# Small routing tables in bfloat16 instead of float32, and the first one-hot columns made in two halves

## The chip, the core and the metric

The kernel runs on one NeuronCore of one Trainium2 chip. The metric is the device time of one execution in microseconds (us), the median over several executions.

## The reference

Three stages follow each other, all on float32 data.

```python
# 1. retention attention: q, k, v of shape (4, 8, 768, 64)
gamma = 1.0 - 2.0 ** (-5.0 - np.arange(H))
for t in range(S):
    state = gamma[None, :, None, None] * state + np.einsum('bhd,bhe->bhde', k[:, :, t], v[:, :, t])
    y[:, :, t] = scale * np.einsum('bhd,bhde->bhe', q[:, :, t], state)
x = y.transpose(0, 2, 1, 3).reshape(3072, 512)

# 2. mixture of 8 experts, each takes exactly 384 tokens
logits = x @ w_gate                            # (3072, 8)
order = np.argsort(-logits.flatten())          # all (token, expert) pairs, highest first
for idx in order:
    tok, e = int(idx) // E, int(idx) % E
    if assigned[tok] >= 0 or counts[e] >= cap: continue
    assigned[tok] = e
    counts[e] += 1
out[mask] = np.maximum(x[mask] @ w1[e], 0.0) @ w2[e]     # for each e, mask = assigned == e

# 3. gated layer with d_ff = 1536
gate = 1.0 / (1.0 + np.exp(-(x @ w_gate2)))
return gate * (x @ w_val) @ w_out
```

## The kernel before, in words

**The order of the work.** The attention runs first, over 24 units of 128 tokens (`attend_*`, 0 to about 131 us). In the same time SyncE (SP) loads q, k and v, stores the finished rows to a buffer `xrows` in DRAM, and begins to load the weights of the third stage that stay in SBUF (`resident`). Each matrix product of stages 2 and 3 is made of three float32r products (high x high, high x low, low x high), so each weight piece is split in a high part (ScalarE) and a low part (VectorE or GpSimd) before use.

**The routing.** It assigns tokens to experts without a sort. Each partition holds 24 tokens (U = 24) and 8 experts (E = 8), so a table over both has 192 columns. VectorE (the DVE) takes for each token its best open expert (`prepare_keys`, `prepare_digits`: `best`, `wide`, `top`, `choice`), turns the logit into an integer key of 7 digits of 5 bits, and then finds digit by digit the key down to which the fullest expert is filled. Every step is a "visit": VectorE writes a small table, TensorE multiplies it with a table of ones or a triangle to sum over partitions, and VectorE reads the sum back (`route(vis, i)` on VectorE, `visit(vis, i)` on TensorE). Visits 1 to 7 are digits (`compare_first`, L981, in the first round; `compare`, L991, in the others). `V_TIE` (L1080 to L1088) counts ties, `V_COUNT` (L1091 to L1101) says which of them fit, `V_RANK` (L1104 to L1117) finds the filled expert and its members, `V_IDS` (L1121 to L1124) their ranks. `make_onehot` (L1133, L1135) writes for each token a one-hot row `onehot` (32 columns by the low rank bits) and a row `slot_ids` (24 columns) that carries the token's number in the block of its rank. TensorE multiplies them (L1355, 24 matmuls in the first round), which turns them into the list of token numbers, `route_ids` (L1163) writes it to `ids`, and GpSimd gathers the 384 rows of x from DRAM (L839) in three thirds.

**Tables and how they are read.** The two operands of an operation on a 192-column table come as `[P, E, U]`. `per_token(ap)` repeats a 24-column table over the experts (the outer dimension has step 0, the inner one has step 1); `per_expert(ap)` repeats an 8-column table over the tokens (the inner dimension has step 0). `over_experts(ap)` turns the order to `[P, U, E]`, so a reduction over the inner dimension steps by 24 elements.

**Which of the routing is in the open.** The routing for the first expert, round 0, stands alone between the attention and the first expert's products: nothing else is left for TensorE. All instructions of VectorE follow each other there (`link` makes the next one wait for the last). After the first ids `close` and `prepare(False)` begin the second routing, then VectorE splits 4 weight pieces of `ring` (L1211) and the low part of x (L1192). TensorE runs 44 matmuls without use (`keep_busy`, L1367) while the gather is under way, transposes x (L1375), and the main loop begins with L1382. The routing of round i + 1 is laid into the products of round i: TensorE's visits are put by a planner at given columns of the product stream, and VectorE's steps between its other duties.

**Queues.** SP issues all plain transfers in the order of the program: in the attention q, k, v, 4 stores and, now and then, a resident weight; later the late resident weights; after `expert_id` is known (L1113) the 8 ring pieces of the expert (L784). GpSimd issues the gathers (L839) and the final scatters (L853).

**Places in SBUF.** The tables are laid one behind the other in the order of their declaration, each starting at a multiple of 32 bytes in the partition. Behind them comes `resident` at byte 29696, and behind that `ring`, `xh`, `xl`, `hh`, `hl`, `h2h`, `h2l`. The tiles of the attention (`qraw` at byte 115712, `kraw`, `vraw`, `xrow`, ...) are laid over these and move with them. The loads into `qraw`, `kraw` and `vraw` write runs of 256 bytes (64 floats), those into a resident or ring piece of w1, w2, w_gate or w_val runs of 512 bytes.

Of the kernel before, what the change touches and what calls it, by code (L numbers as in the profile page):

```python
# [4 lines left out]
F32 = mybir.dt.float32  # L5
F32R = mybir.dt.float32r
BF16 = mybir.dt.bfloat16
# [3 lines left out]
ALU = mybir.AluOpType  # L11
ACT = mybir.ActivationFunctionType
AX_X = mybir.AxisListType.X
P = 128

def retention_moe_glu_kernel(nc, q, k, v, w_router, w1, w2, w_gate, w_val, w_out, decay, out):
    B, H, S, D = q.shape
    E = w_router.shape[1]
    C = S // P  # L20
    U = B * C
# [11 lines left out]
    with ctx:  # L33
        def sb(name, shape, dt):
            return ctx.enter_context(nc.sbuf_tensor(name, shape, dt))

        def sem(name):
            return ctx.enter_context(nc.semaphore(name))
# [32 lines left out]
        EVACUATED = KF + KD  # L71
# [7 lines left out]
        QUAD = 32  # L79
        QUADS = P // QUAD  # L80
        BLOCKS = CAP // QUAD
# [40 lines left out]
        tied = sb("tied", [P, E, U], BF16)  # L122
        tied_before = sb("tied_before", [P, E, U], BF16)
        fresh = sb("fresh", [P, E, U], BF16)
        wide = sb("wide", [P, E, U], F32)
        best = sb("best", [P, U], F32)
        top = sb("top", [P, 2, U], F32)
        bits = sb("bits", [P, U], F32)
        key = sb("key", [P, U], I32)
        digit_f = sb("digit_f", [P, DIGITS, U], BF16)  # L130
        prefix = sb("prefix", [P, U], BF16)
        is_above = sb("is_above", [P, U], F32)
        is_on = sb("is_on", [P, U], F32)
        fits = sb("fits", [P, U], F32)
        taken = sb("taken", [P, U], F32)
        member = sb("member", [P, U], BF16)
        members_to = sb("members_to", [P, U], F32)
# [2 lines left out]
        rank_low = sb("rank_low", [P, U], I32)  # L140
        rank_block = sb("rank_block", [P, U], I32)
        in_block = sb("in_block", [P, U, BLOCKS], BF16)
        member_id = sb("member_id", [P, U, 2], BF16)
        slot_ids = sb("slot_ids", [P, U, 2, BLOCKS], BF16)
        slot_sums = sb("slot_sums", [P, 2 * BLOCKS], F32)
        room = sb("room", [P, E], F32)
        limit = sb("limit", [P, E], F32)
        filled = sb("filled", [P, E], F32)
        closing = sb("closing", [P, E], F32)
        keeping = sb("keeping", [P, E], F32)  # L150
        numbered = sb("numbered", [P, E], F32)
# [16 lines left out]
        raised = sb("raised", [P, U], F32)  # L168
        shift = sb("shift", [P, DIGITS], I32)
        expert_iota = sb("expert_iota", [P, E], F32)  # L170
        priority = sb("priority", [P, E], F32)
        column = sb("column", [P, QUAD], F32)
        block_iota = sb("block_iota", [P, BLOCKS], F32)
        position = sb("position", [P, U, 2], F32)
# [23 lines left out]
        def placed(name, shape, dt, offset):  # L198
            return nc.alloc_sbuf_tensor_at(name, shape, dt, offset=offset)
# [12 lines left out]
        onehot = placed("onehot", [P, U, QUAD], BF16, at_hl + TT * DM * 4)  # L212
# [14 lines left out]
        onehot_ready = sem("onehot_ready")  # L227
# [22 lines left out]
        h_done = sem("h_done")  # L250
# [697 lines left out]
        def _(dve):  # L948
# [176 lines left out]
                                                 block_iota[:, :].unsqueeze(1).to_broadcast([P, U, BLOCKS]), ALU.is_equal))  # L1125

            def make_onehot(i):
                if not (isinstance(i, int) and i == 0):
                    dve.wait_ge(h_done, EVACUATED * i)
                if isinstance(i, int) and i == 0:  # L1130
                    for c in range(C):
                        dve.wait_ge(xrow_stored[c], STORED * (B + 1))
                nc.vector.tensor_tensor(onehot[:, :, :], column[:, :].unsqueeze(1).to_broadcast([P, U, QUAD]),  # L1133
                                                   rank_low[:, :].unsqueeze(2).to_broadcast([P, U, QUAD]), ALU.is_equal).then_inc(onehot_ready, 1)
                nc.vector.tensor_tensor(slot_ids[:, :, :, :], in_block[:, :, :].unsqueeze(2).to_broadcast([P, U, 2, BLOCKS]),  # L1135
                                        member_id[:, :, :].unsqueeze(3).to_broadcast([P, U, 2, BLOCKS]), ALU.mult).then_inc(onehot_ready, 1)

            def close():

# [172 lines left out]
        def _(pe):  # L1312
# [4 lines left out]
            def visit(vis, i):  # L1317
                if vis < V_TIE:

                    for t in range(0, U, FOLD):  # L1320
                        if t == 0:
                            pe.wait_ge(half_compared, i * DIGITS + vis + 1)
                        if t == U // 2:
                            pe.wait_ge(route_ready, i * (VISITS - 1) + vis + 1)
                        if isinstance(i, int) and i == 0:
                            bins = above_first[:, t // FOLD, :, :].rearrange("p r t -> p (r t)")
                        else:
                            bins = above[:, t:t + FOLD, :].rearrange("p t r -> p (t r)")
                        last = nc.tensor.matmul(PS_R[:, 0:FOLD * E], bins, choice[:, :, t:t + FOLD], start=t == 0, stop=t == U - FOLD)  # L1329
                    last.then_inc(route_done, 1)  # L1330
                    if isinstance(i, int) and i == 0:
                        pe.wait_ge(partial_ready, vis + 1)
                        for t in range(FOLD):
                            last = nc.tensor.matmul(PS_K[:, 0:E], fold[:, t, :, :].rearrange("p k r -> p (k r)"), partial[:, :, t],
                                                    start=t == 0, stop=t == FOLD - 1)
                        last.then_inc(folded, 1)
                    return
                if vis < V_IDS:
                    pe.wait_ge(route_ready, i * (VISITS - 1) + vis + 1)
                if vis == V_TIE:  # L1340

                    nc.tensor.matmul(PS_R[:, 0:NF], below[:, :], tied[:, :, :].rearrange("p e u -> p (e u)"), start=True, stop=False)
                    nc.tensor.matmul(PS_R[:, 0:NF], ones[:, :], tied_before[:, :, :].rearrange("p e u -> p (e u)"), start=False, stop=True)
                    last = nc.tensor.matmul(PS_K[:, 0:E], ones[:, :], counted[:, :], start=True, stop=True)
                elif vis == V_COUNT:
                    last = nc.tensor.matmul(PS_K[:, 0:E], ones[:, :], counted_fresh[:, :], start=True, stop=True)
                elif vis == V_RANK:

                    nc.tensor.matmul(PS_K[:, 0:U], below[:, :], member[:, :], start=True, stop=False)
                    last = nc.tensor.matmul(PS_K[:, 0:U], ones[:, :], members_before[:, :], start=False, stop=True)  # L1350
                else:
                    pe.wait_ge(onehot_ready, 2 * (i + 1))
                    if isinstance(i, int) and i == 0:
                        for t in range(U):
                            last = nc.tensor.matmul(PS_R[0:QUAD, 0:2 * BLOCKS], onehot[:, t, :],  # L1355
                                                    slot_ids[:, t, :, :].rearrange("p n m -> p (n m)"), start=t == 0, stop=t == U - 1)
                    else:
                        for t in range(0, U, QUADS):
                            last = nc.tensor.matmul(PS_R[:, 0:QUADS * 2 * BLOCKS], onehot[:, t:t + QUADS, :].rearrange("p t c -> p (t c)"),
                                                    slot_ids[:, t:t + QUADS, :, :].rearrange("p t n m -> p (t n m)"),  # L1360
                                                    start=t == 0, stop=t == U - QUADS)
                last.then_inc(route_done, 1)
# [170 lines left out]
```

## Time and profile before

| | us |
|---|---|
| median of 3 executions | 1074.85 (1074.79 to 1075.24) |
| the profiled execution | 1075.28 |
| its span | 1073.5 |
| TensorE busy (matmuls) | 1029.4 (96%) |
| VectorE busy | 704.0 (66%) |
| ScalarE busy | 326.2 (30%) |
| GpSimd busy | 122.6 (11%) |
| mean granted TensorE clock | 0.979 |

The span is the time from the first to the last recorded instruction or transfer of the profiled execution; 1.8 us lie around it. Busy shares are averages over stages with different limits, so they have to be read by stage: the attention (0 to 131 us), the routing of the first expert in the open (131 to 174 us), the main loop (174 to 1062 us) and the last rows on their way out (1062 to 1073.5 us).

### The profile page before, as it was taken

What the parts mean: (1) busy time and instruction counts of PE and PEld (TensorE: products, weight loads), DVE (VectorE), ACT (ScalarE), POOL (GpSimd) and SP (SyncE); (2) the same over time, 40 slices, a digit from 0 to 9 for tenths busy, and PEclk for the clock granted to TensorE, in tenths of its full rate; (3) what the DMA queues carried; (4) which work ended last, traced back from release to release, by engine and by line L of the source; (5) the groups of instructions that cost most, each with busy time, mean ns of one, the idle gap of its engine ahead of it and who ended that gap; (6) DMA issues with size and microseconds to landing.
All of it is one profiled execution on the core that took longest, in us unless ns stands there. A gap on an engine that the chain in (4) does not pass through costs nothing.

```text
span 1073.5 us, 20171 instructions
## 1 busy us (share of the span) xinstructions
PE 1029.4 (96%) x7186; PEld 960.5 (89%) x7186; DVE 704.0 (66%) x1880; ACT 326.2 (30%) x622; POOL 122.6 (11%) x149
## 2 busy tenths in 40 slices
PE   8999728999999999999999999999999999999995
PEld 7888618989999999999999999999999999999995
DVE  4777778788678657765776577667765677554211
ACT  3222144412342234223332333223322341334110
POOL 4323301045200110010101010001001100110001
PEclk9999958999999999999999999999999999999998
DMA  9989765304230414132413232233214231423000
GB/s 204 211 211 224 170 201 155 111 4 140 77 116 21 128 55 134 39 89 79 131 58 89 79 119 70 61 106 109 80 48 120 89 99 40 128 70 117 2 1 29
DMA packets 197356, 107.69 MB, mean 100 GB/s; under 512 B 81936, under 2 KB 182800, under 8 KB 197264
## 3 DMA queue, kind: packets, MB, share of 16 engines
q1 hardware_dynamic: 193424, 93.94, 31.6%
q0 software_dynamic: 3840, 12.59, 3.7%
q8 instruction: 50, 0.82, 0.3%
q14 instruction: 42, 0.34, 0.1%
HBM read 88.41 MB, written 18.09 MB: 99 GB/s over the span
## 4 chain that ended last, share of the span: by engine, by line
PE 95%; DVE 3%; issue 1%; DMA 1%; POOL 0%; DVEq 0%; ACT 0%; POOLq 0%
PE bank L1382 21%; PE bank L1384 21%; PE bank L1383 21%; PE bank L1475 6%; PE bank L1476 6%; PE bank L1474 6%; PE bank L660 2%; PE bank L730 2%; PE bank L726 2%; PE bank L686 1%; PE bank L1329 1%; PE bank L693 1%; PE bank L740 1%; PE bank L638 1%; PE bank L707 1%
## 5 line engine op out<-in xcount | busy, mean ns | idle before, releaser
L1382 PE MATMUL bank<-h2h,resident 128*128 128x384 f32 x768 | 261.2, 340 | 0.0
L1384 PE MATMUL bank<-h2h,resident 128*128 128x384 f32 x768 | 257.9, 336 | 0.0
L1383 PE MATMUL bank<-h2l,resident 128*128 128x384 f32 x768 | 257.3, 335 | 0.0
L1382 PEld LDWEIGHTS bank<-h2h,resident 128*128 128x128 f32 x768 | 144.3, 188 | 2.9
L1383 PEld LDWEIGHTS bank<-h2l,resident 128*128 128x128 f32 x768 | 144.3, 188 | 2.9
L1384 PEld LDWEIGHTS bank<-h2h,resident 128*128 128x128 f32 x768 | 144.1, 188 | 0.0
L885 ACT ACTIVATE ring<-ring_raw 128x512 fp32r<-128x512 f32 x192 | 117.7, 623 | 54.7 <-DMA ring_raw<-in_moe_w_out_dram 43.1
L1202 DVE TENSOR_TENSOR pf<-bank,gate 128x384 f32<-128x384 f32 x96 | 53.5, 557 | 116.0 <-PE bank L1384 108.1
L1211 DVE TENSOR_TENSOR ring<-ring_raw,ring 128x512 fp32r<-128x512 f32 x192 | 128.7, 696 | 0.0
L909 ACT ACTIVATE ph<-pf 128x384 fp32r<-128x384 f32 x96 | 50.4, 525 | 257.5 <-DVE pf L1202 257.5
L1206 DVE TENSOR_TENSOR pl<-pf,ph 128x384 fp32r<-128x384 f32 x96 | 55.4, 577 | 56.8 <-ACT ph L909 56.8
L905 ACT ACTIVATE gate<-bank 128x384 f32<-128x384 f32 x96 | 46.9, 489 | 141.2 <-PE bank L1384 141.1
L1382 PE MATMUL bank<-xh,ring 128*128 128x384 f32 x256 | 87.6, 342 | 0.9 <-DVE xl L1192 0.9
L1382 PE MATMUL bank<-hh,ring 128*128 128x384 f32 x256 | 87.0, 340 | 0.0
L1384 PE MATMUL bank<-xh,ring 128*128 128x384 f32 x256 | 85.7, 335 | 0.0
L1383 PE MATMUL bank<-hl,ring 128*128 128x384 f32 x256 | 85.7, 335 | 0.0
L1384 PE MATMUL bank<-hh,ring 128*128 128x384 f32 x256 | 85.7, 335 | 0.0
L1383 PE MATMUL bank<-xl,ring 128*128 128x384 f32 x256 | 85.7, 335 | 0.0
L1476 PE MATMUL bank<-ring,pl 128*128 128x512 f32 x192 | 76.0, 396 | 0.0
L1475 PE MATMUL bank<-ring,ph 128*128 128x512 f32 x192 | 75.8, 395 | 0.0
L839 POOL DMA_INDIRECT xg<-xrows,ids x24 | 23.7, 989 | 455.4 <-DVE ids L1163 417.2
L1474 PE MATMUL bank<-ring,ph 128*128 128x512 f32 x192 | 74.8, 390 | 0.2 <-issue 0.2
(195 smaller groups left out, 1660.2 us busy)
## 6 DMA issues: line engine op xcount, KB each, us to landing
ring_raw<-in_moe_w_dram SPq DMA_DIRECT2D x128, 256.0 KB, 3.1
ring_raw<-in_moe_w_out_dram SPq DMA_DIRECT2D x64, 256.0 KB, 2.9
qraw<-in_q_dram SPq DMA_DIRECT2D x24, 256.0 KB, 4.1
kraw<-in_k_dram SPq DMA_DIRECT2D x24, 256.0 KB, 4.3
vraw<-in_v_dram SPq DMA_DIRECT2D x24, 256.0 KB, 4.4
xrows<-xrow SPq DMA_DIRECT2D x96, 64.0 KB, 2.1
xlaid<-xg SPq DMA_DIRECT2D x7, 768.0 KB, 4.5
zg<-xlaid SPq DMA_DIRECT2D x28, 192.0 KB, 4.2
```

Of the source, the lines that this page charges most:

```text
L885: nc.scalar.activation(ring[:, n % RING, 0, :], ring_raw[n % RING][:, :], ACT.Copy).then_inc(piece_hi, 1)
L905: nc.scalar.activation(gate[:, f % 2, :], bank[2 * (f % 2)][:, 0:CAP], ACT.Sigmoid).then_inc(gate_ready, 1)
L909: nc.scalar.activation(ph[:, f % 2, :], pf[:, f % 2, :], ACT.Copy).then_inc(ph_ready, 1)
L1202: nc.vector.tensor_tensor(pf[:, f % 2, :], bank[2 * (f % 2) + 1][:, 0:CAP], gate[:, f % 2, :], ALU.mult).then_inc(p_ready, 1)
L1206: nc.vector.tensor_tensor(pl[:, f % 2, :], pf[:, f % 2, :], ph[:, f % 2, :].bitcast(F32), ALU.subtract).then_inc(pl_ready, 1)
L1211: nc.vector.tensor_tensor(ring[:, s, 1, :], ring_raw[s][:, :], ring[:, s, 0, :].bitcast(F32), ALU.subtract).then_inc(piece_lo, 1)
L1382: nc.tensor.matmul(ps, wh, xhi, start=start, stop=False)
L1383: nc.tensor.matmul(ps, wh, xlo, start=False, stop=False)
L1384: return nc.tensor.matmul(ps, wl, xhi, start=False, stop=stop)
L1474: nc.tensor.matmul(PS_OUT[j][:, :], ph[:, f % 2, toks], wh, start=f == 0, stop=False)
L1475: nc.tensor.matmul(PS_OUT[j][:, :], ph[:, f % 2, toks], wl, start=False, stop=False)
L1476: last = nc.tensor.matmul(PS_OUT[j][:, :], pl[:, f % 2, toks], wh, start=False, stop=False)
```

## The change

Seven tables change their type from float32 to bfloat16: `wide` (192 columns), `top` (48), `is_above`, `is_on`, `fits` (24 each), `filled` and `priority` (8 each). All of them hold whole numbers up to 24 (flags, priorities 8 to 1, counts up to 24), which bfloat16 holds exactly. `make_onehot` of the first round (`i == 0`) writes tokens 0 to 11 and then tokens 12 to 23, each half with its own pair of instructions and its own increments of `onehot_ready`; TensorE starts its first 12 matmuls after the first pair and waits again before the 13th. For the other rounds the instructions are as before, and the count that TensorE waits for is 2 higher, since the first round now increments four times.

```diff
@@ -122,16 +122,16 @@
         tied = sb("tied", [P, E, U], BF16)
         tied_before = sb("tied_before", [P, E, U], BF16)
         fresh = sb("fresh", [P, E, U], BF16)
-        wide = sb("wide", [P, E, U], F32)
+        wide = sb("wide", [P, E, U], BF16)
         best = sb("best", [P, U], F32)
-        top = sb("top", [P, 2, U], F32)
+        top = sb("top", [P, 2, U], BF16)
         bits = sb("bits", [P, U], F32)
         key = sb("key", [P, U], I32)
         digit_f = sb("digit_f", [P, DIGITS, U], BF16)
         prefix = sb("prefix", [P, U], BF16)
-        is_above = sb("is_above", [P, U], F32)
-        is_on = sb("is_on", [P, U], F32)
-        fits = sb("fits", [P, U], F32)
+        is_above = sb("is_above", [P, U], BF16)
+        is_on = sb("is_on", [P, U], BF16)
+        fits = sb("fits", [P, U], BF16)
         taken = sb("taken", [P, U], F32)
         member = sb("member", [P, U], BF16)
         members_to = sb("members_to", [P, U], F32)
@@ -145,7 +145,7 @@
         slot_sums = sb("slot_sums", [P, 2 * BLOCKS], F32)
         room = sb("room", [P, E], F32)
         limit = sb("limit", [P, E], F32)
-        filled = sb("filled", [P, E], F32)
+        filled = sb("filled", [P, E], BF16)
         closing = sb("closing", [P, E], F32)
         keeping = sb("keeping", [P, E], F32)
         numbered = sb("numbered", [P, E], F32)
@@ -168,7 +168,7 @@
         raised = sb("raised", [P, U], F32)
         shift = sb("shift", [P, DIGITS], I32)
         expert_iota = sb("expert_iota", [P, E], F32)
-        priority = sb("priority", [P, E], F32)
+        priority = sb("priority", [P, E], BF16)
         column = sb("column", [P, QUAD], F32)
         block_iota = sb("block_iota", [P, BLOCKS], F32)
         position = sb("position", [P, U, 2], F32)
@@ -1125,15 +1125,20 @@
                                                  block_iota[:, :].unsqueeze(1).to_broadcast([P, U, BLOCKS]), ALU.is_equal))
 
             def make_onehot(i):
-                if not (isinstance(i, int) and i == 0):
-                    dve.wait_ge(h_done, EVACUATED * i)
                 if isinstance(i, int) and i == 0:
                     for c in range(C):
                         dve.wait_ge(xrow_stored[c], STORED * (B + 1))
-                nc.vector.tensor_tensor(onehot[:, :, :], column[:, :].unsqueeze(1).to_broadcast([P, U, QUAD]),
-                                                   rank_low[:, :].unsqueeze(2).to_broadcast([P, U, QUAD]), ALU.is_equal).then_inc(onehot_ready, 1)
-                nc.vector.tensor_tensor(slot_ids[:, :, :, :], in_block[:, :, :].unsqueeze(2).to_broadcast([P, U, 2, BLOCKS]),
-                                        member_id[:, :, :].unsqueeze(3).to_broadcast([P, U, 2, BLOCKS]), ALU.mult).then_inc(onehot_ready, 1)
+                    parts = 2
+                else:
+                    dve.wait_ge(h_done, EVACUATED * i)
+                    parts = 1
+                n = U // parts
+                for part in range(parts):
+                    tiles = slice(part * n, part * n + n)
+                    nc.vector.tensor_tensor(onehot[:, tiles, :], column[:, :].unsqueeze(1).to_broadcast([P, n, QUAD]),
+                                            rank_low[:, tiles].unsqueeze(2).to_broadcast([P, n, QUAD]), ALU.is_equal).then_inc(onehot_ready, 1)
+                    nc.vector.tensor_tensor(slot_ids[:, tiles, :, :], in_block[:, tiles, :].unsqueeze(2).to_broadcast([P, n, 2, BLOCKS]),
+                                            member_id[:, tiles, :].unsqueeze(3).to_broadcast([P, n, 2, BLOCKS]), ALU.mult).then_inc(onehot_ready, 1)
 
             def close():
 
@@ -1349,9 +1354,11 @@
                     nc.tensor.matmul(PS_K[:, 0:U], below[:, :], member[:, :], start=True, stop=False)
                     last = nc.tensor.matmul(PS_K[:, 0:U], ones[:, :], members_before[:, :], start=False, stop=True)
                 else:
-                    pe.wait_ge(onehot_ready, 2 * (i + 1))
+                    pe.wait_ge(onehot_ready, 2 if i == 0 else 2 * (i + 2))
                     if isinstance(i, int) and i == 0:
                         for t in range(U):
+                            if t == U // 2:
+                                pe.wait_ge(onehot_ready, 4)
                             last = nc.tensor.matmul(PS_R[0:QUAD, 0:2 * BLOCKS], onehot[:, t, :],
                                                     slot_ids[:, t, :, :].rearrange("p n m -> p (n m)"), start=t == 0, stop=t == U - 1)
                     else:
```

By the rule of 32 bytes, `wide` takes 384 bytes less in a partition, `top` 96 less, `is_above`, `is_on` and `fits` 32 less each (48 bytes are rounded to 64), `filled` and `priority` nothing less. Everything behind them, from `resident` on, starts 576 bytes earlier.

## Rows read from the trace of the kernel before

**Rows 1.** The chain that ended last, its shares of the span by engine.

```profile
PE 95%; DVE 3%; issue 1%; DMA 1%; POOL 0%; DVEq 0%; ACT 0%; POOLq 0%
```

**Rows 2.** Stretches: length; PE, PEld, DVE, ACT, POOL busy; granted clock; DMA share; GB/s.

```profile
80.50:107.00 26.50, 26.50 (x416) 23.13 (x414) 21.05 (x39) 7.42 (x18) 8.70 (x9) 1.00 0.96 226
...
167.00:168.00 1.00, 1.00 (x8) 0.95 (x7) 0.93 (x5) 0.72 (x2) 0.70 (x1) 0.50 1.11 334
...
600.00:800.00 200.00, 200.00 (x1165) 188.81 (x1164) 137.01 (x393) 63.53 (x118) 8.99 (x10) 1.00 0.28 84
```

**Rows 3.** What TensorE waited for from 176 us on: us, times, longest.

```profile
PE bank L1474 <- issue: 0.2, 1, 0.2
```

**Rows 4.** Timeline, first routing: start us, us, engine, line, operation, shapes, [idle before].

```profile
133.48 0.61 DVE L1043 TENSOR_REDUCE top<-wide 128x24 f32<-128x192 f32 x1
...
152.41 0.36 DVE L1082 TENSOR_TENSOR tied<-choice,is_on 128x192 bf16<-128x192 bf16 x1
...
153.28 0.33 DVE L1085 TENSOR_TENSOR strict<-choice,is_above 128x192 bf16<-128x192 bf16 x1
...
153.65 0.35 DVE L1087 TENSOR_REDUCE counted<-strict 128x8 bf16<-128x192 bf16 x1
153.92 0.35 DVE L1088 TENSOR_TENSOR tied_before<-wide,tied 128x192 bf16<-128x192 f32 x1
...
155.46 0.62 DVE L1094 TENSOR_REDUCE fits<-wide 128x24 f32<-128x192 f32 x1
156.11 0.36 DVE L1095 TENSOR_TENSOR fresh<-tied,fits 128x192 bf16<-128x192 bf16 x1
156.50 0.26 DVE L1096 TENSOR_TENSOR fresh<-fresh,strict 128x192 bf16<-128x192 bf16 x1
...
157.35 0.48 DVE L1100 TENSOR_REDUCE taken<-fresh 128x24 f32<-128x192 bf16 x1
...
159.03 0.61 DVE L1109 TENSOR_REDUCE member<-wide 128x24 bf16<-128x192 f32 x1
159.67 0.15 DVE L1113 CAST expert_id<-expert_f 128x1 int32<-128x1 f32 x1
...
161.24 4.94 SPq L784 DMA_DIRECT2D ring_raw<-in_moe_w_dram  x8
161.49 0.96 DVE L1133 TENSOR_TENSOR onehot<-column,rank_low 128x768 bf16<-128x768 f32 x1
162.36 0.75 DVE L1135 TENSOR_TENSOR slot_ids<-in_block,member_id 128x576 bf16<-128x576 bf16 x1
163.17 0.81 PE L1355 MATMUL bank<-slot_ids,onehot 128*32 128x24 bf16 x24 [2.73 <-DVE slot_ids L1135]
```

**Rows 5.** Groups by line and form, DVE: xcount, busy us, mean ns, idle before.

```profile
L991 DVE TENSOR_TENSOR above<-prefix,ladder 128x384 bf16<-128x384 bf16 x84 | 43.2, 555 | 1.5
...
L981 DVE TENSOR_TENSOR above_first<-prefix,ladder 128x384 bf16<-128x384 bf16 x12 | 3.8, 355 | 0.2
```

**Rows 6.** The chain from the ids to the main loop: start us, us, what.

```profile
165.76 4.95 DMA xg<-xrows,ids
...
173.18 0.50 ACT xh L890
...
173.71 0.57 DVE xl L1192
```

**Rows 7.** Timeline: first load of the attention, then k of the last unit.

```profile
1.25 0.42 SPq L376 DMA_DIRECT2D qraw<-in_q_dram  x1
...
111.12 1.04 POOL L480 TENSOR_TENSOR ks<-kraw,dec 128x512 f32<-128x512 f32 x1 [0.63 <-DMA kraw<-in_k_dram]
...
115.77 0.60 PE L693 MATMUL bank<-ident,ks 128*128 128x128 f32 x4
```

**Rows 8.** Timeline beside the gather: `keep_busy` and the splits of four weight pieces.

```profile
163.91 6.29 PE L1367 MATMUL bank<-segment,ones 128*128 128x192 bf16 x44
...
170.76 2.49 DVE L1211 TENSOR_TENSOR ring<-ring_raw,ring 128x512 fp32r<-128x512 f32 x4
```

## The prediction, made before the changed kernel was run

> **What bounds the kernel now.** I read the chain of waits first. TensorE holds 95% of the chain that ended last, VectorE 3% [rows 1]. The stretches say where each applies: in the attention TensorE is busy for the whole of 26.5 us, in the main loop for 200 of 200 us [rows 2]. The waits confirm the loop: from 176 us on TensorE waited 0.2 us in all [rows 3]. VectorE is busy for 137 of 200 us there [rows 2], and none of its routing ends late. So whatever the change saves in the routings of the seven later experts is worth nothing, and it must be judged on the routing of the first one, which lies in the open between the attention and L1382.
>
> The timeline of that stretch is a single line of VectorE instructions, each waiting for the last, with short visits to TensorE between them [rows 4]. There a nanosecond off an instruction is a nanosecond off the start of the main loop, as long as nothing else becomes late. From the ids on the chain is the gather (4.95 us from the first issue to landing), the transposes, ScalarE's `xh` and VectorE's `xl` [rows 6].
>
> **Part 1, element by element.** Which of the tables gain is read from three rows. `fresh <- fresh,strict`, all bfloat16 with inner step 1, takes 0.26 us for 192 columns; `fresh <- tied,fits`, the same but for a float32 `fits`, takes 0.36 [rows 4]. `tied_before`, with one float32 operand, takes 0.35. So one float32 operand costs the fast rate. What a step of 0 does is seen in the two compares of 384 columns: `above_first`, whose inner run has step 1 and whose step of 0 lies further out, takes 355 ns, and `above`, whose inner step on an operand is 0, takes 555 ns [rows 5]. A table repeated over the outer dimension keeps the fast rate, one repeated over the inner does not.
>
> In the changed kernel `tied` and `strict` (through `per_token`), `tied_before` and `fresh <- tied,fits` become all bfloat16 with inner step 1. I set each at 0.26 us: `tied` 0.36 to 0.26, `strict` 0.33 to 0.26, `tied_before` 0.35 to 0.26, `fresh` 0.36 to 0.26 [rows 4]. Sum 0.10 + 0.07 + 0.09 + 0.10 = 0.36 us. Lower bound 0.09 (only `tied_before`, where nothing is repeated), if the repetition over the experts does spoil the rate; upper bound 0.40. The other writes of `wide` keep a float32 operand or a PSUM source, or they use `per_expert` (`priority`, `filled`) with inner step 0: nothing. `is_on`, `is_above` and `filled` are of 24 and 8 columns, where the fixed part is nearly all of the time: nothing, at most 0.02 us each either way. The scan that writes `wide` goes column after column already on bfloat16 operands: nothing.
>
> **Part 2, reductions.** `top`, `fits` and `member` reduce `wide` over the experts, stepping by 24 elements, in 0.61, 0.62 and 0.61 us. `taken` reduces a bfloat16 table in the same order in 0.48 us, and `counted` reduces as many columns with step 1 in 0.35 us [rows 4]. `taken` is an addition and the three are a maximum and a minimum, so the 0.13 us between them may be the type (a step of 48 bytes in place of 96) or the operation. I take the type, since maximum and minimum agree with each other and the step is what divides `counted` from `taken`: 0.13 + 0.14 + 0.13 = 0.40 us. Bounds: 0 if it is the operation; 0.26 + 0.27 + 0.26 = 0.79 if they fell to `counted`.
>
> The Trainium skill ("VectorE: DVE Perf Modes", The perf-mode tier table) puts `tensor_reduce` at one element per cycle for bfloat16 and float32 alike. Taken alone that gives the reductions nothing and a whole change of 0.6 us in place of 1.0. The rows do show reductions of 192 columns at 0.35, 0.48 and 0.61 us, so something beside the count of columns sets their time here.
>
> **Part 3, the two halves.** Before: `onehot` starts at 161.49, `slot_ids` at 162.36, that is 0.87 us later for 768 columns, and ends at 163.11; TensorE starts at 163.17 and needs 0.81 us for 24 matmuls [rows 4]. The slope is (0.96 - 0.555) / 384, about 1.05 ns a column, from `onehot` and from `above` with 384 columns [rows 4, 5], so 0.40 us for 384 columns and 0.80 for 768, with 0.155 fixed, of which 0.07 remain when the next instruction needs no wait (0.87 - 0.80). Two halves then start at 161.49, 161.49 + 0.40 + 0.07 = 161.96, + 0.30 + 0.07 = 162.33, + 0.47 = 162.80, and the last ends after 0.30 + 0.15 at 163.25. TensorE's first 12 matmuls start at 162.47 and are over near 162.9, hidden under VectorE's second half. The other 12 start at 163.31 and take 0.43 us (half of 0.81 and a little for the start), to 163.74, where it was 163.98 before. Gain 0.24 us. The half costs VectorE 0.14 us (two more instructions) and saves 0.38 on TensorE. The bounds are -0.14 (the matmuls pass nothing on) and 0.38 (the extra instructions cost nothing). The second wait stands ahead of matmul 13; behind it are the last matmuls and `keep_busy`, which nobody waits for.
>
> **Sum and what is late next.** Up to `expert_id` the chain shortens by 0.36 + 0.40 = 0.76 us, up to the ids by 1.00 us. Behind that:
> - SP issues the 8 ring pieces after `expert_id` (161.24 before, so 160.5) and GpSimd the gather after the ids (165.76, so 164.8). Both use the transfer engines, which are full while they run (share 1.11 at 334 GB/s in [rows 2]). The gather moves 1.00 us, the pieces that it competes with only 0.76. Its landing should move by something between; I take 0.9.
> - `keep_busy` ended at 163.91 + 6.29 = 170.20, 0.5 us before the first third was there (170.71) [rows 6, 8]. It moves by 1.0 too, so it stays in cover, and TensorE's granted clock (0.50 in [rows 2], the level of 1.2 GHz) rises as far into it as before.
> - VectorE's four splits ended at 170.76 + 2.49 = 173.25, and `xh` was there at 173.68 [rows 6, 8]: 0.43 us of slack. They move by 1.0 and by another 0.13 from `top` in the second preparation.
>
> So 0.9 us. The profiled execution took 1075.28 us, 1.8 more than its span of 1073.5, and 0.43 more than the median. It becomes 1074.4, and the median 1074.85 becomes **1073.95 us**. All three parts without loss in the gather give 1073.85; with the upper bounds of parts 1 and 2 and 0.24 for the halves 1.43, hence 1073.4.
>
> **Edits of place.** Everything from `resident` on starts 576 bytes earlier. It began at a multiple of 512 and will begin 448 past one, so each 256-byte run of q, k and v that was written from a multiple of 256 begins 192 past one. No row of before shows loads with such a start. Cost taken: nothing; the bound on the bad side is the third rival.
>
> **Rivals.**
> 1. *The type does little.* The step of 0 keeps `tied`, `strict` and `fresh` at one rate and the reductions are slow by their operation. Left are `tied_before` and the halves, 0.09 + 0.24 = 0.33 us: 1074.5. For it: no row shows `per_token` on all-bfloat16 operands, and `taken` differs in its operation. Against it: `above_first` at 355 ns.
> 2. *The gather is bound by the transfers in front of it.* Then its landing moves with the pieces only, 0.76 us: 1074.1. For it: the full share of 1.11. Against it: the first third is the first of three to ask for its bandwidth and gets it beside the pieces.
> 3. *Slower: the loads of the attention take longer at their new places.* The place is k of the last unit. It landed at 111.12, GpSimd was done with it at 112.16, and TensorE took it at 115.77 [rows 7]: 3.6 us of slack, the end of loads that SP began to issue at 1.25 us [rows 7] and that share the engines at 0.96 [rows 2]. Loads longer by more than 3.6 / 109.9 = 3.3% make TensorE wait. If they took 10% longer, the attention would end 11.0 - 3.6 = 7.4 us later, less the 0.9: 1081.3. For it: the share of 0.96, and that the slack is only 3% of the stretch. Against it: TensorE never waited for these loads before, and the bytes are the same.
>
> **How the numbers follow.** Forecast (0.6 to 1.3 us, the second rival inside it, of which it has 0.2): 0.67. First rival: 0.14. Third: 0.08. A gain of over 2.15 us by the new places, which I can't derive: 0.05. Something else within 0.2%: 0.06. What a measurement of this kernel tells from no change is about 0.2%, 2.15 us, 1072.7 to 1077.0. The forecast, both small rivals and the rest lie inside, so faster 0.05, same 0.86, slower 0.09. The range of 8 in 10 takes the forecast, the first rival and a part of the rest: 1073.0 to 1075.4.
>
> **What the new profile would show.** `tied`, `strict`, `tied_before` and `fresh <- tied,fits` at 0.26 us; `top`, `fits` and `member` near 0.48 (at 0.61 part 2 is wrong, and the operation was the cause); `onehot` and `slot_ids` twice at about 0.55 and 0.45, L1355 in two groups of 12, the second ending about 2.25 us after the first `onehot` began (2.49 before); `expert_id` 0.76 us and L1382 0.9 us earlier against the end of the attention. The end of the attention unmoved says that the third rival is out. The forecast fails if TensorE waits for `ks` or `qraw` before 120 us, or if the main loop, from L1382 to the last L1466, differs in length by more than 0.3 us.

## The result and the profile after

The changed kernel is slower. Its median over 19 executions is 1077.13 us (1075.58 to 1078.92), that of the kernel before, run beside it, 1075.21 (1074.28 to 1076.17). The ratio is 1.0018, 95% interval 1.0012 to 1.0024. The forecast was 1073.95 with a range up to 1075.4. What the change does to instructions came out close to the forecast; the loss came from where the large tiles lie. The profiled execution took 1078.59 us, its span is 1076.8, 3.3 more than that of before.

The timeline of the first routing after the change (columns as in [rows 4]):

```profile
133.89 0.47 DVE L1043 TENSOR_REDUCE top<-wide 128x24 bf16<-128x192 bf16 x1
...
152.66 0.26 DVE L1082 TENSOR_TENSOR tied<-choice,is_on 128x192 bf16<-128x192 bf16 x1
...
153.43 0.23 DVE L1085 TENSOR_TENSOR strict<-choice,is_above 128x192 bf16<-128x192 bf16 x1
...
153.97 0.25 DVE L1088 TENSOR_TENSOR tied_before<-wide,tied 128x192 bf16<-128x192 bf16 x1
...
155.41 0.48 DVE L1094 TENSOR_REDUCE fits<-wide 128x24 bf16<-128x192 bf16 x1
155.92 0.26 DVE L1095 TENSOR_TENSOR fresh<-tied,fits 128x192 bf16<-128x192 bf16 x1
...
158.73 0.47 DVE L1109 TENSOR_REDUCE member<-wide 128x24 bf16<-128x192 bf16 x1
...
161.05 0.56 DVE L1138 TENSOR_TENSOR onehot<-column,rank_low 128x384 bf16<-128x384 f32 x1
...
162.36 0.45 DVE L1140 TENSOR_TENSOR slot_ids<-in_block,member_id 128x288 bf16<-128x288 bf16 x1
162.87 0.50 PE L1362 MATMUL bank<-slot_ids,onehot 128*32 128x24 bf16 x12 [0.34 <-DVE slot_ids L1140]
163.30 5.17 PE L1374 MATMUL bank<-segment,ones 128*128 128x192 bf16 x44
```

Each of these lines answers to one of [rows 4] and is about as short as forecast; only L1362's second group took 0.50 us where 0.43 was forecast. From the start of `best` (131.63 before, 132.19 after) to the first gather (165.76 and 165.16) VectorE's chain took 34.13 us before and 32.97 after, 1.16 us less. Of these, 0.14 us are not the change's: `bits` took 0.32 us in the profile of before, where it ran beside a subtraction on GpSimd, and 0.18 us here. That leaves 1.02 us, for 1.00 forecast.

What came against it stands in three other views. First the stretch from 5 to 105 us (columns as in [rows 2]) of before, and then of after:

```profile
5.00:105.00 100.00, 100.00 (x1547) 88.04 (x1543) 71.91 (x127) 27.59 (x63) 33.78 (x49) 1.00 0.94 218
```

```profile
5.00:105.00 100.00, 98.48 (x1540) 86.36 (x1538) 71.62 (x126) 27.72 (x63) 33.82 (x49) 1.00 1.05 215
```

And the transfers of the hardware queue over the whole span (packets, MB, share of 16 engines' time), of before and of after:

```profile
q1 hardware_dynamic: 193424, 93.94, 31.6%
```

```profile
q1 hardware_dynamic: 193424, 93.94, 33.8%
```

Same packets and bytes, more engine time: per packet 0.316 x 16 x 1073.5 / 193,424 = 28.1 ns before and 30.1 ns after, and in the attention a share of 1.05 for 215 GB/s where 0.94 carried 218, 13% more time a byte. TensorE, never idle there before, now waits. Second, that wait, in the timeline of after:

```profile
9.89 1.04 POOL L480 TENSOR_TENSOR ks<-kraw,dec 128x512 f32<-128x512 f32 x1 [2.94 <-DMA kraw<-in_k_dram]
...
10.99 0.66 PE L693 MATMUL bank<-ident,ks 128*128 128x128 f32 x4 [1.28 <-POOL ks L480]
...
112.15 1.04 POOL L480 TENSOR_TENSOR ks<-kraw,dec 128x512 f32<-128x512 f32 x1 [0.47 <-DMA kraw<-in_k_dram]
...
116.33 0.60 PE L693 MATMUL bank<-ident,ks 128*128 128x128 f32 x4
```

These are the longest wait, at the second unit, and k of the last unit. The start of the attention in before (the first 48 matmuls, then k of the second and of the third unit), and then in after (the 48 matmuls, k of the third and of the fourth unit):

```profile
2.92 5.39 PE L638 MATMUL bank<-ident,dec 128*64 128x128 f32 x48 [2.92 <-DMA dec<-in_decay_dram]
...
10.95 0.60 PE L693 MATMUL bank<-ident,ks 128*128 128x128 f32 x4
...
14.09 0.60 PE L693 MATMUL bank<-ident,ks 128*128 128x128 f32 x4
```

```profile
2.85 4.23 PE L638 MATMUL bank<-ident,dec 128*64 128x128 f32 x48 [2.85 <-DMA dec<-in_decay_dram]
...
14.59 0.66 PE L693 MATMUL bank<-ident,ks 128*128 128x128 f32 x4 [0.24 <-POOL ks L480]
...
19.28 0.60 PE L693 MATMUL bank<-ident,ks 128*128 128x128 f32 x4
```

The wait of 1.28 us is not what is lost. TensorE takes k of the second unit at 10.99 us, at 10.95 in before; it stood ready earlier, because its first 48 matmuls took 4.23 us in this execution and 5.39 in the other. The loss comes right behind: the third unit is 0.50 us later than before (14.59 for 14.09), the fourth 0.56 (19.28 for 18.72), and it stays 0.56 to the last. At the last unit 3.1 us of slack are left, nearly the 3.6 of [rows 7]. Third, the gather in the chain of waits (start us, us), then TensorE's timeline behind it, then the stretches by the microsecond:

```profile
165.16 6.40 DMA xg<-xrows,ids
```

```profile
171.60 0.75 PE L1382 MATMUL bank<-ident,xg 128*128 128x128 f32 x4 [3.13 <-DMA xg<-xrows,ids]
...
175.99 0.66 PE L1389 MATMUL bank<-xh,ring 128*128 128x384 f32 x1 [0.62 <-DVE xl L1197]
```

```profile
170.00:171.00 1.00, 0.00 (x0) 0.00 (x0) 1.00 (x4) 0.73 (x2) 0.00 (x0) 1.00 1.06 388
...
173.00:174.00 1.00, 1.00 (x8) 0.91 (x8) 0.00 (x0) 0.00 (x0) 0.00 (x0) 0.50 0.00 0
...
178.00:179.00 1.00, 1.00 (x9) 0.95 (x9) 1.00 (x3) 0.00 (x0) 0.00 (x0) 0.50 0.08 16
```

The gather lands 6.40 us after its issue, 4.95 before [rows 6]. TensorE had run out of `keep_busy` at 168.47 and idled for 3.13 us (0.56 before); some 1.5 us after it resumed the granted clock was at 0.50 (1.2 GHz), and stayed there past 178 us.

The 3.3 us of span add up by these marks: end of the attention +0.56, VectorE's chain -1.16, issue of the gather to the first transpose +1.44, from there to the first product +0.74 (3.65 to 4.39, half the clock), main loop +1.68 (887.75 to 889.43 between the first product and the last `orow`, half the clock at its start), tail +0.04.

### The profile page after: what moved, and what is told of

It reads as the page before. It is cut to its first block, busy times and chain, and to the rows that moved or that the text cites. A ratio compares the mean times of both kernels' runs of the same rounds, so it can differ in the third digit from the quotient of the medians.

```text
span 1076.8 us, 20173 instructions
## 1 busy us (share of the span) xinstructions
PE 1030.3 (96%) x7186; PEld 960.7 (89%) x7186; DVE 697.5 (65%) x1882; ACT 326.7 (30%) x622; POOL 122.3 (11%) x149
## 3 DMA queue, kind: packets, MB, share of 16 engines
q1 hardware_dynamic: 193424, 93.94, 33.8%
## 4 chain that ended last, share of the span: by engine, by line
PE 94%; DVE 3%; DMA 1%; issue 1%; SPq 1%; POOL 0%; DVEq 0%; ACT 0%; POOLq 0%
PE bank L1389 21%; PE bank L1391 21%; PE bank L1390 21%; PE bank L1482 6%; PE bank L1483 6%; PE bank L1481 6%; PE bank L660 2%; PE bank L730 2%; PE bank L726 2%; PE bank L1334 1%; PE bank L686 1%; PE bank L693 1%; PE bank L740 1%; PE bank L707 1%; DMA xg<-xrows,ids 1%
```

## The experiments

Theory P: the 576 bytes that the smaller tables free shift every large tile off a multiple of 256 bytes, and the transfers that write or read them take longer. Rivals: C, the halves start TensorE earlier and `keep_busy` no longer covers the gather; B, the bfloat16 tables cost something themselves. Every comparison is with the kernel before, run on the same chip (medians 1075.21 to 1075.28).

**The places alone.** To the changed kernel, or to the kernel before, one unused table is added behind the small ones:

```diff
+        room_left = sb("room_left", [P, 16], F32)    # a_even: changed kernel, resident at 29184, a multiple of 512
+        room_left = sb("room_left", [P, 112], F32)   # b_odd: kernel before, resident at 30144, 448 past one
         at_above = nc.sbuf_base
```

> The changed kernel with 64 unused bytes behind the tables, so that resident and everything behind it begin at a multiple of 512 bytes again (29184), as in the kernel before (29696); after has 29120. Theory P (places): the slower kernel comes from transfers that write and read tiles at 448 past a multiple of 512. Then the transfer share of the hardware queue falls from 33.8% back to 31.6%, TensorE no longer waits for ks (1.5 us in after), the first third of the gather lands about 5.0 us after its issue (6.4 in after), and the time is 1073.8 to 1074.6, 1.2 to 0.6 under before. Theory C (cover): the first half of the one-hot columns starts TensorE 1.1 us earlier, its clock rises earlier, the 44 keep_busy matmuls run out in 5.2 instead of 6.3 us, TensorE idles and its clock falls before the main loop. Then the gap and the fall stay in part of the executions whatever the places: some of them at about 1073.9 and others at about 1076. Theory B (bfloat16 tables cost something by themselves): the time stays at 1077.

> The kernel before with 448 unused bytes behind the tables: no other edit, all large tiles begin 448 past a multiple of 512, as in after. Theory P: transfer share of the hardware queue near 33.8% (31.6 before), TensorE waits 0.5 to 1.5 us for ks in the attention, the gather's first third lands 6 us after its issue instead of 5, so TensorE idles some 1.5 us behind keep_busy instead of 0.6, and the time is 1.0 to 3.5 us above before. Theory C or B: as before, within 0.3 us.

a_even: 1074.41 us (11 executions, 1073.49 to 1077.59), ratio 0.9995 (0.9986 to 1.0004). b_odd: 1077.94 us (8, 1076.86 to 1079.02), ratio 1.0026 (1.0015 to 1.0036). The same stretch and the gather in the chain, first of a_even (hardware queue 31.8%), then of b_odd (33.8%):

```profile
5.00:105.00 100.00, 100.00 (x1550) 88.02 (x1547) 72.53 (x128) 27.46 (x63) 34.80 (x50) 1.00 0.95 220
```

```profile
164.05 5.25 DMA xg<-xrows,ids
```

```profile
5.00:105.00 100.00, 99.53 (x1538) 87.26 (x1536) 71.44 (x126) 27.59 (x63) 33.87 (x49) 1.00 1.04 213
```

```profile
166.39 6.23 DMA xg<-xrows,ids
```

With no other edit, the kernel before becomes 2.7 us slower by an unused table, with the share and the gather of after and a wait for `ks` of 0.5 us (1.5 in after). The changed kernel is brought from 1.9 us over before to 0.8 under it. P holds; B falls. That a_even is faster than before is not shown by its times, since the interval includes 1.

In the profile of b_odd the clock did not fall (1.00 from 169 to 180 us), though TensorE was idle for 2.42 us ahead of the transposes:

```profile
172.66 0.75 PE L1376 MATMUL bank<-ident,xg 128*128 128x128 f32 x4 [2.42 <-DMA xg<-xrows,ids]
```

So it shows the cost of the places without the clock. Its span is 2.2 us longer than that of before: end of the attention +0.54, VectorE's chain +0.09, issue of the gather to the first transpose +1.27 (6.27 for 5.00), from there to the first product nothing (3.65), main loop +0.23 (887.98 for 887.75), tail +0.07.

**The two edits apart**, both with the tiles at a multiple of 512:

```diff
-                    parts = 2       # types_even: the changed tables and 64 unused bytes, one-hot columns in one piece
+                    parts = 1
-        wide = sb("wide", [P, E, U], BF16)   # halves_only: wide and the six other tables in float32
+        wide = sb("wide", [P, E, U], F32)
```

> The seven tables in bfloat16, one-hot columns in one piece as before, large tiles at a multiple of 512. By the durations seen in after (best to expert_id) 0.9 us less VectorE time ahead of the gather; keep_busy starts with the ids as before, so TensorE idles no longer than before. All theories but B: 0.6 to 0.9 us under before, and no spread wider than that of before. B: slower than before.

> Only the first one-hot columns in two halves, tables in float32, places as before. The ids come 0.25 us earlier. Theory C: TensorE starts 0.7 us earlier, the clock may rise a step earlier and keep_busy ends up to 1.3 us earlier, so that TensorE idles 1 to 2 us ahead of the first transposes and the clock falls in some executions: the times lie in two groups about 2.4 us apart, the lower 0.25 us under before. Theory P or B: 0.2 us under before, in one group.

types_even: 1074.22 us (1073.81 to 1077.13), 1.0 under before, ratio 0.9993 (0.9984 to 1.0002). halves_only: 1075.15 (1074.83 to 1075.64), ratio 1.0000 (0.9991 to 1.0009). A gain of 0.2 us is less than these intervals can tell; none shows, and types_even without the halves is no slower than a_even with them (1074.41). In the profile of halves_only the first gather was issued 33.80 us after `best` began, 0.33 earlier than before (0.14 of it is `bits` again), and the first transpose came 5.39 us after that, 0.39 later than before. This is what my second rival would give, but it is not shown: the same stretch took 5.42 us in b_256 (below), which has the gather, the instructions and the alignment of before, so that it moves as much from one execution to the next. C as I put it falls: `keep_busy` took 6.29 us in halves_only, as before, and 4.96 in types_even, where the halves are not. When the clock rises in it differs from one execution to the next.

**The fall of the clock.** The changed kernel with its tiles misplaced, and with them in place, with a longer cover:

```diff
-            keep_busy(44)
+            keep_busy(60)     # a_busy60: places of the changed kernel
+            keep_busy(50)     # a_even_busy50: with the 64 unused bytes of a_even
```

> The changed kernel with its tiles where they are (448 past a multiple of 512), keep_busy(60) in place of keep_busy(44). The profile of after has TensorE idle for 3.1 us between keep_busy and the first third of x, then the granted clock at 0.5 from about 173 to 178 us, which costs some 2.4 us against before in the transposes and the first products. The 19 times of after lie between 1075.6 and 1078.9, 8 of them under 1076.5. Theory D (the fall of the clock behind a gap is what spreads them, on top of the places): without the gap all times lie at 1075.6 to 1076.6, median 1076.1. Theory E (the spread is that of the transfers alone): median and spread as in after, 1077.1 and 1075.6 to 1078.9.

> The changed kernel with 64 unused bytes behind the tables and keep_busy(50) in place of 44: both costs taken away. Expected 1074.2 to 1074.4, 0.8 to 1.0 under before, and no time at 1077 (a_even had one at 1077.6 in 11). If the longer keep_busy itself runs past the landing of x, 1074.6 to 1075.0.

a_busy60: 1076.04 us (1075.71 to 1077.18), ratio 1.0008 (0.9999 to 1.0017); its granted clock was 1.00 from 171 to 180 us. Of the 19 times of the changed kernel 10 are above 1077, of these 11 one. That one is the profiled execution, in which the clock did not fall. So the longer cover takes most of the slow executions away, 1.1 us between the medians (1077.13 - 1076.04). How much of this is the clock's fall is not shown. In the profile of after it cost 2.4 us (0.74 + 1.68 above). Its 6.6 us at half the clock take 0.003 off the mean granted clock of an execution, which is 0.982 at the most in any run. Of the ten executions above 1077 four have a mean of 0.978 and two of 0.979, but four have 0.980 or 0.981, which hardly leaves room for such a fall, and the median one (1077.13, 0.980) is one of these. By this the clock fell in some six of 19 at the most, and something else makes others slow. Nor does every gap bring a fall: in the profiles it came behind gaps of 3.13 us (after) and 2.49 (a_attn_even, below), and not behind 2.44 (b_32), 2.42 (b_odd), 2.16 (b_64) and 2.14 (types_even). What is left in a_busy60, 0.8 us over before, is at the edge of what these executions tell from nothing. a_even_busy50: 1074.12 (1073.85 to 1075.10), ratio 0.9993 (0.9984 to 1.0002), without the single time at 1077 that a_even and types_even had.

**Which tiles.** Only the attention's tiles moved back, or only ring and what lies behind it:

```diff
-        shared = at_big + (RESIDENT - SHARED) * 2 * 512 * 4
+        shared = at_big + (RESIDENT - SHARED) * 2 * 512 * 4 + 64   # a_attn_even
+        room_left = sb("room_left", [P, 16], F32)                  # a_ring_even
         at_ring = nc.sbuf_base
```

> The changed kernel with only the tiles of the attention moved 64 bytes on, so that qraw, kraw and vraw begin at a multiple of 512; resident, ring and xg stay at 448 past one. Theory F (the place costs mostly in the attention): the attention ends as before, TensorE does not wait for ks, and the time is near that of a_even, 1074.4 to 1075.0. Theory G (it costs mostly in the first round, where resident, ring and gather share the engines): the share of the attention falls to that of before, the gather still lands in 6 us and the time is 1076 to 1077.

> The changed kernel with 64 unused bytes between resident and ring: ring, xg and all behind them begin at a multiple of 512; resident and the tiles of the attention stay at 448 past one. Theory F: the attention still ends some 0.5 us late and the time stays above 1076. Theory G: the first third of the gather lands within 5.2 us, the times lie at 1074.6 to 1075.2 and are no more spread than those of before.

a_attn_even: 1075.29 us (1074.47 to 1077.57), ratio 1.0002 (0.9993 to 1.0011). The share from 5 to 105 us is 0.95 at 221 GB/s, TensorE does not wait for `ks`, but the first transpose follows the gather's issue by 5.81 us, and in 2 of 11 the time is over 1077. a_ring_even: 1074.83 (1073.17 to 1076.92), ratio 0.9995 (0.9986 to 1.0004). Its share is 1.05 at 216 GB/s and it waits for `ks`; that stretch takes 5.34 us. Each half cures its own stage, so both theories are half right; the 5.81 us of a_attn_even lie between the 5.00 to 5.53 of the kernels with every tile in place and the 6.15 to 6.44 of those with none, so the attention's tiles may have a part in the gather too.

The wait for `ks` alone is a poor sign of the places: a_even_busy50 and a_split_busy50 (below) wait 0.74 and 0.76 us at the second unit with the attention's tiles in place, and their first 48 matmuls took 4.14 and 4.34 us. What goes with the places in all profiles is the time from k of the second unit to k of the third on TensorE: 3.60 to 3.62 us in the six kernels with the attention's tiles off a multiple of 256, 3.13 to 3.20 in the eight with them on one. TensorE took k of the last unit at 116.17 to 116.43 us in the six and at 115.05 to 115.77 in the eight.

Two things were not expected. GpSimd's last split of a resident weight ran into the first routing (it began at 131.37 us in after, behind loads that landed earlier); timeline of a_ring_even:

```profile
132.88 1.27 POOL L279 TENSOR_TENSOR resident<-resident_raw,resident 128x512 fp32r<-128x512 f32 x1
132.94 1.43 DVE L1035 TENSOR_TENSOR wide<-logits,best 128x192 bf16<-128x192 f32 x1
```

VectorE's 0.35 us instruction takes 1.43 and ends 0.2 us after GpSimd's. A like hold stands in the profiles of a_busy60 and b_64, where `key` takes 1.12 us in place of 0.18, and not in that of after. And the rounds of the main loop were shorter in a_ring_even than in any kernel so far. The start of `orow` in two rounds that follow each other, first a_even, then a_ring_even:

```profile
507.26 1.89 DVE L1223 COPY orow<-bank 128x512 f32<-128x512 f32 x3 [1.96 <-PE bank L1474]
618.56 1.89 DVE L1223 COPY orow<-bank 128x512 f32<-128x512 f32 x3 [1.96 <-PE bank L1474]
```

```profile
508.97 1.89 DVE L1223 COPY orow<-bank 128x512 f32<-128x512 f32 x3 [2.02 <-PE bank L1474]
620.05 1.89 DVE L1223 COPY orow<-bank 128x512 f32<-128x512 f32 x3 [2.02 <-PE bank L1474]
```

111.30 us and 111.08, and so in every round.

**The version that these point to, and the grid of places.** The two edits of a_attn_even and a_ring_even together with `keep_busy(50)`, which leaves only `resident` off a multiple of 256; and the kernel before with 256, 64 and 32 unused bytes in front of the large tiles:

```diff
+        room_left = sb("room_left", [P, 64], F32)    # b_256; b_64: [P, 16]; b_32: [P, 8]
         at_above = nc.sbuf_base
```

> The changed kernel with keep_busy(50), the tiles of the attention and ring, xg and all behind them at a multiple of 512, and only resident still 448 past one. a_ring_even showed rounds of the main loop of 111.08 us in place of 111.29, 1.5 us over the loop, all of it gained in the gate and value products; its attention ended late. Theory R (the loop's 0.2 us a round comes with resident and ring at different places modulo 512): rounds of 111.08 us here too, and with the attention in place the time is 1.5 us under a_even_busy50: 1072.5 to 1073.0. Theory S (it is one execution's chance): rounds of 111.29 and 1074.1.

> The kernel before with 256 unused bytes behind the tables: all large tiles 256 past a multiple of 512. Theory 256 (only the rest modulo 256 counts): share of the transfer engines from 5 to 105 us 0.94 as in before, 1075.2. Theory 512: share 1.04 and 1077 as in b_odd.

> The kernel before with 64 unused bytes behind the tables: all large tiles 64 past a multiple of 512, still a multiple of 64. Theory 256: slower as b_odd (448 past one is 192 past a multiple of 256), share 1.04 from 5 to 105 us, 1076.5 to 1078. Theory 64 (another cause in b_odd, not the crossing of 256 bytes): as before.

> The kernel before with 32 unused bytes behind the tables: all large tiles 32 past a multiple of 512, no multiple of 64. Theory 256: as b_64, 1076.5 to 1078. Theory of finer steps (a write that does not begin at a multiple of 64 costs more again): share over 1.1 from 5 to 105 us and over 1079.

a_split_busy50: 1072.90 us (1072.29 to 1073.40), ratio 0.9979 (0.9970 to 0.9988), 2.3 us under before, the fastest of all and the only one of the runs whose interval lies under 1. Its rounds take 111.08 to 111.14 us. b_256: 1075.61 (1074.76 to 1076.71), ratio 1.0004 (0.9995 to 1.0013). b_64: 1077.53 (1076.76 to 1079.71), ratio 1.0024 (1.0014 to 1.0033). b_32: 1078.08 (6 executions, 1076.86 to 1079.41), ratio 1.0027 (1.0015 to 1.0039). The stretch from 5 to 105 us of b_256, b_64 and b_32:

```profile
5.00:105.00 100.00, 100.00 (x1545) 87.84 (x1541) 72.11 (x127) 27.40 (x63) 34.83 (x50) 1.00 0.95 222
```

```profile
5.00:105.00 100.00, 98.45 (x1540) 86.28 (x1538) 71.64 (x127) 27.55 (x63) 33.81 (x49) 1.00 1.04 213
```

```profile
5.00:105.00 100.00, 99.44 (x1536) 87.08 (x1534) 71.31 (x126) 27.69 (x63) 33.81 (x49) 1.00 1.05 215
```

A start at a multiple of 256 is as good as one at a multiple of 512; 32, 64 and 448 past one cost the same share, so it matters whether a start is off the boundary and not how far. That the boundary is 256 bytes and not 128 is not shown: no kernel here has its tiles at an odd multiple of 128. The Trainium skill's account ("DMA: Bandwidth & Descriptors", How a descriptor splits into AXI transactions) has a boundary of 256 bytes. Its account of a start off the boundary would give the attention's 256-byte runs two transactions for one; the runs show 13% more engine time a byte there, much less than double. (It does not give every such start one transaction more, as the prediction put it: the Trainium skill's 96-byte example has one either way.)

## Why the prediction was wrong

*What bounds the kernel* was right for the instructions: VectorE's chain in the open stretch was the one to shorten, and it became 1.02 us shorter. It left out the attention, which b_odd shows to count too (+0.54 us).

*Part 1* held: 0.10, 0.10, 0.10 and 0.10 us, 0.40 in all, where 0.36 were forecast. A step of 0 on the outer dimension keeps the fast rate, one on the inner does not (`wide <- wide,priority` all in bfloat16 still takes 0.35).

*Part 2* held: 0.61, 0.62 and 0.61 became 0.47, 0.48 and 0.47. The type was the cause and not the operation: maximum and minimum now run at the 0.48 of the addition. By the Trainium skill's one rate for both types ("VectorE: DVE Perf Modes", The perf-mode tier table) they would not have moved; the measurement decides against it for this strided form.

*Part 3* was right in its instructions and wrong in its worth. TensorE ended 2.32 us after the first `onehot` began, for 2.49 before and 2.25 forecast. So they saved 0.17 us for 0.24 forecast, since TensorE's second group took 0.50 us for 0.43. In the times the halves show nothing (halves_only 1075.15 for 1075.21), which is no finer than these times can tell.

*Sum and what is late next* failed at `keep_busy` and at the gather. The gather was to land 0.9 us earlier; it took 6.40 us from its issue for 4.95 and landed at 171.56 us for 170.71. By the places alone the first transpose came 1.27 us later behind the issue (b_odd). I wrote that it "stays in cover" and that the clock "rises as far into it as before". It took 6.29 us in one profiled execution, and I took that for its length; the runs show 4.96 to 6.45 for the same 44 matmuls, according to when the clock rises. With a late gather it leaves a gap up to 3.1 us, behind which the clock fell in the profiled execution and in some five of the other 18 at the most.

*Edits of place* is the step that turned the sign. I counted the 576 bytes, saw the 192 past a multiple of 256, and set "Cost taken: nothing". The shift costs 2.7 us, by b_odd against before and by the changed kernel against a_even. In b_odd's profile 2.2 us come without any fall of the clock; what part the fall has in the median of the changed kernel stays open.

*The third rival* had the right cause at 8% and the wrong place. I priced it at the last unit, where 3.6 us of slack were to be used up. The loads there still were in time. By its price, 13% more on 109.9 us less the slack of 3.6 would have cost over 10 us; the attention ended 0.56 us later, and of the slack 3.1 us were left. The engines were busier by a share of 1.05 for 0.94, but carried nearly the same bytes (215 GB/s for 218). The loss arose where no slack had been measured: between the second and the third unit, in the gather behind eight ring pieces, and, in some executions, in GpSimd's split that runs into VectorE's routing. The threshold of 3.3% said nothing on these. Both signs that the prediction named for its own failure came: TensorE waited for `ks`, and the main loop grew by more than 0.3 us (1.68).

## What to carry to other kernels

A table that shrinks moves everything declared behind it: after any edit of sizes, compare the start of every tile that transfers write, modulo 256, before and after, and pad the tables so that the large tiles keep their place. A slack read at the end of a stretch does not cover its start, where the first loads have none. A wait is not a loss by itself: compare the time at which the work starts, since the engine may only have arrived earlier. A filler that keeps TensorE's clock up must be sized for the execution in which the clock rises first, since it then runs out earliest.

## What the hardware showed that was not expected

- The transfers' time depends on whether the tile in SBUF starts at a multiple of 256 bytes (0 and 256 modulo 512 against 32, 64 and 448; 128 was not run): 28.1 ns a packet at 0 and 30.1 at 448 past a multiple of 512 (before and after, mean packet 486 bytes), 13% more engine time a byte in the attention.
- A bfloat16 reduction of 192 columns in steps of 24 elements takes 0.47 to 0.48 us, in float32 0.61 to 0.62, and with step 1 in bfloat16 0.35.
- An instruction of VectorE that met GpSimd's 1.27 us subtraction took 1.43 us in place of 0.35 and ended 0.2 us after it. Not every one is held: in b_64 `wide` took its usual 0.35 us beside GpSimd's subtraction, and `key` behind it 1.12 in place of 0.18. No run isolates it.
- With `resident` at 448 and `ring` at 0 modulo 512 a round takes 0.2 us less (111.08 to 111.14) than with both at the same place (a_even, b_odd and all others: 111.28 to 111.32). The gate and value products give it. What in the access makes the difference stays open; two kernels show it, some 1.5 us over the loop in the profiles, and 1.2 us between the medians of a_split_busy50 and a_even_busy50.
